# Expert tiles turned round: tokens held stationary for the first tile of a one-tile expert and for a third tile

## The reference

```python
# 1. recurrent attention over 768 steps -> x, 1536 tokens of 384
# 2. h = x @ w_in (384x2048); g = max(h,0) + alpha*min(h,0); x = g @ w_out
# 3. experts: N = 1536, D = 384, E = 8, F = 1024
logits = x @ w_gate
expert_idx = np.argmax(logits, axis=1)
...
disp = np.zeros((E, capacity, D), dtype=np.float32)   # capacity 384
...
h = np.maximum(np.einsum('ecd,edf->ecf', disp, w1), 0.0)
y = np.einsum('ecf,efd->ecd', h, w2)
...
out[i] = gate_w[i] * y[expert_idx[i], pos[i]]
```

## Time and profile before

| | |
|---|---|
| median of 3 runs | 450.17 us (448.96 to 450.79) |
| the profiled execution's own time | 451.07 us |
| its span, first to last instruction | 449.2 us |
| PE busy | 423.4 us, 94% of the span |
| DVE / ACT / POOL busy | 259.4 / 197.1 / 176.4 us |
| mean granted TensorE clock | 0.983 of full speed |
| mean DMA traffic | 137 GB/s |

### The profile page before, as it was taken

One profiled execution on the slowest core, in us unless ns is written; L12 is line 12 of the kernel. 1 busy time (PEld: TensorE's weight loads), 2 busy tenths in 40 slices (PEclk: granted clock), 3 DMA queues, 4 the chain that ended last, 5 costly groups with the idle time before them and its releaser, 6 DMA issues.

```text
span 449.2 us, 9383 instructions
## 1 busy us (share of the span) xinstructions
PE 423.4 (94%) x3333; PEld 409.6 (91%) x3333; DVE 259.4 (58%) x555; ACT 197.1 (44%) x450; POOL 176.4 (39%) x189
## 2 busy tenths in 40 slices
PE   6799999999999999999999986699999999998893
PEld 5688889999999999999999985599999999998893
DVE  6798867775435333633437663444578684648820
ACT  2789943432311122111323332334568684548721
POOL 4999616553323532244535851420110311011112
PEclk9899999999999999999999998989999999999997
DMA  7996034537950000000013440683676866564000
GB/s 251 403 337 193 3 112 141 154 88 254 367 217 19 35 1 0 0 35 18 0 35 91 139 140 17 227 307 92 207 218 197 262 190 204 158 211 110 10 19 7
DMA packets 33935, 61.45 MB, mean 137 GB/s; under 512 B 4654, under 2 KB 26910, under 8 KB 33888
## 3 DMA queue, kind: packets, MB, share of 16 engines
q1 hardware_dynamic: 31008, 55.53, 38.4%
q0 software_dynamic: 2880, 5.29, 3.4%
HBM read 47.53 MB, written 14.79 MB: 139 GB/s over the span
## 4 chain that ended last, share of the span: by engine, by line
PE 79%; DVE 7%; ACT 5%; issue 3%; POOL 2%; DMA 2%; POOLq 0%; SPq 0%; DVEq 0%; ACTq 0%
PE bank L1150 20%; PE bank L1165 19%; PE bank L1275 18%; PE bank L1304 14%; ACT scores L611 3%; PE bank L1262 2%; PE bank L1119 1%; PE bank L1083 1%; ACT w_high L594 1%; DVE scores L826 1%; DMA xe<-routed_rows 1%; DVE neg L884 1%; DVE act_full L890 1%; PE bank L1111 1%; PE bank L1069 1%
## 5 line engine op out<-in xcount | busy, mean ns | idle before, releaser
L510 POOL TENSOR_TENSOR g_low<-act_full,g_high 128x384 fp32r<-128x384 f32 x63 | 63.8, 1012 | 114.5 <-ACT g_high L640 114.5
L640 ACT ACTIVATE g_high<-act_full 128x384 fp32r<-128x384 f32 x64 | 33.7, 526 | 150.0 <-DVE act_full L890 137.3
L1150 PE MATMUL bank<-x_split,w_high 128*128 (+1 forms) x384 | 98.4, 337 | 0.0
L884 DVE TENSOR_SCALAR neg<-bank,alpha_sb 128x384 f32<-128x384 f32 x64 | 39.2, 613 | 71.5 <-PE bank L1150 71.4
L566 POOL DMA_INDIRECT out<-y_out,token x24 | 25.2, 1049 | 124.6 <-ACT y_out L727 123.4
L1150 PEld LDWEIGHTS bank<-x_split,w_high 128*128 128x128 f32 x384 | 69.0, 188 | 0.2 <-issue 0.2
L1165 PE MATMUL bank<-w_high,g_high 128*128 128x384 f32 x189 | 65.1, 344 | 1.2 <-POOL g_low L510 1.2
L1150 PE MATMUL bank<-x_split,w_low 128*128 (+1 forms) x192 | 64.4, 336 | 0.0
L1165 PE MATMUL bank<-w_high,g_low 128*128 128x384 f32 x189 | 63.8, 337 | 0.0
L1165 PE MATMUL bank<-w_low,g_high 128*128 128x384 f32 x189 | 63.7, 337 | 0.0
L1275 PE MATMUL bank<-xe_high,w_high 128*128 128x256 f32 (+1 forms) x192 | 58.8, 306 | 1.6 <-DVE xe_low L1003 1.6
(11 more groups left out here) (127 smaller groups left out, 796.2 us busy)
## 6 DMA issues: line engine op xcount, KB each, us to landing
w_raw<-chunks SPq DMA_DIRECT2D x96, 192.0 KB, 3.3
w_raw<-chunks SPq DMA_DIRECT2D x32, 384.0 KB, 3.2
rk_in<-att_rk SPq DMA_DIRECT2D x12, 704.0 KB, 6.3
routed_rows<-fill SPq DMA_DIRECT2D x1, 5211.0 KB, 17.3
xe<-routed_rows SPq DMA_DIRECT2D x7, 579.0 KB, 5.5
v_in<-att_v SPq DMA_DIRECT2D x12, 200.0 KB, 5.5
out<-fill SPq DMA_DIRECT2D x1, 2304.0 KB, 23.4
x_split<-x_split POOLq DMA_DIRECT2D x18, 48.0 KB, 2.6
```

The lines of the kernel that those rows point to most:

```text
L510: pool.tensor_tensor(gl[:, f % 4, :], act_full[:, f % 2, :], gh[:, f % 4, :].bitcast(f32), ALU.subtract).then_inc(s_gl, 1)
L640: act.activation(gh[:, f % 4, :], act_full[:, f % 2, :], ACT.Copy).then_inc(s_gh, 1)
L884: dve.tensor_scalar(neg[:, f % 2, :], h, 0.0, alpha_sb[:, f:f + 1], ALU.min, ALU.mult)\
L1150: last = mm(bank[f % 4][:, 0:G], a[:, f, w], x[:, kc, bass.ds(g * G, G)], start=kc == 0 and i == 0, stop=kc == KC - 1 and i == 2)
```

## The change

An expert now has two branches of its own on PE and one on ACT and DVE.

- *One tile* (`rows[e] < P + 1`): `flip_up` holds the tile of tokens stationary and streams four weight blocks at once, 9 matmuls of 512 columns for half of the hidden units, into bank 0 or 1. `flip_relu` (DVE) writes the maximum with 0 into the new buffer `gn`, `flip_turn` (PE) transposes it block by block into bank 2 or 3, `flip_high` (ACT) and `flip_low` (DVE) make `egh` and `egl`. The turns of the next expert's three tiles stand between the two halves.
- *Otherwise*: up with 256 columns, then down of tile 1.
- *A third tile*: `flip_up` and so on for tile 2 alone, between the halves of tile 0's down part; its down part comes last.
- DVE and ACT run `flip_relu`, `flip_high` and `flip_low` for tile 2 in every expert, also where there is none; PE then has released them in advance. PE's next use of banks 0 to 3 waits for them (`flip_banks_free`).
- The second halves of the weights are split in one run behind the up part; the output tiles are copied in the order 1, 2, 0 (`Y_ORDER`), tile 0 behind all eight splits of first halves.
- Expert 0 starts with two turned tiles; the third is turned after block 1. Chunks 29 to 31 are split between its blocks. SP waits for expert 0's rows before it issues further loads.

```diff
@@ -417,6 +426,8 @@
             sp.wait_ge(s_scat, 16 * T)
             for i in range(GT):
                 sp.dma_start(xe[:, 0, i, :], disp[i * P:(i + 1) * P, :]).then_inc(s_xe0[i], 16)
+            for i in range(GT):
+                sp.wait_ge(s_xe0[i], 16)
             for m in range(DEFER, RAW):
                 load_chunk(2 * NF - RAW + m, m)
             load_xe(1)
...
-                pool.wait_ge(s_yo, e * GT + GT - i + C_YO)
+                pool.wait_ge(s_yo, e * GT + Y_ORDER.index(i) + 1 + C_YO)
...
+            for e in range(E):
+                for i in Y_ORDER:
+                    y_scatter(e, i, s_out if e < E - 1 else s_last)
+                if e < E - 1:
+
+                    pool.wait_ge(s_out, (e + 1) * 16 * GT)
+                    pool.sem_inc(s_gone, 1)
...
-                act.wait_ge(s_mh, (e - FIRST) * NFE + f + 1)
+                act.wait_ge(s_w1free, e - FIRST + 1)
...
-            for i in range(GT):
+            for i in range(GT - 1):
                 xe_high(0, i, bank[4 + i])
-            for c in range(2 * NF - 3, 2 * NF):
-                split_high(c)
...
+            def flip_high(e, i):
+
+                act.wait_ge(s_step, e * NFE + FFN_STEPS)
+                act.wait_ge(s_yd[2], e)
+                for half in range(2):
+                    act.wait_ge(s_ft[i // 2], 2 * e + half + 1)
+                    if i:
+                        act.wait_ge(s_mgl, e * NFE + NFE + C_MGL)
+                    act.activation(egh[:, half * HF:(half + 1) * HF, i * P:(i + 1) * P],
+                                   bank[2 + half][:, :].rearrange("p (f n) -> p f n", f=HF), ACT.Copy)\
+                       .then_inc(s_fc[i // 2], 1)
+
+            for e in range(E):
+                with act.If(rows[e] < P + 1):
...
+                    if e < E - 1:
+                        for i in range(GT):
+                            xe_high(e + 1, i, bank[4 + GT - 1 - i])
+                    flip_high(e, 0)
+                    act.sem_inc(s_mgh, NFE)
+                with act.Else():
+                    act.sem_inc(s_fc[0], 2)
+                    for f in range(NFE):
+                        relu(e, f, 2 * P)
+                        if e == 0 and f == 1:
+                            xe_high(0, 2, bank[6])
+                        if e == 0 and 3 <= f < 6:
+                            split_high(2 * NF - 6 + f)
+                        if f in TURN and e < E - 1:
+                            xe_high(e + 1, TURN[f], bank[4 + GT - 1 - TURN[f]])
+                if FIRST <= e + 1 < E:
+                    for f in range(NFE):
                         split_high2(e + 1, f)
-
-            for e in range(E):
-                with act.If(rows[e] < 2 * P + 1):
-                    ups(e, 2 * P)
-                with act.Else():
-                    ups(e, CAP)
+                y_copy(e, 1)
+                flip_high(e, 2)
                 for f in range(NFE):
                     if e + FIRST < E:
                         split_high1(e + FIRST, f)
-                    if f in (3, 5, 7):
-                        y_copy(e, (7 - f) // 2)
+                    if f == HF:
+                        y_copy(e, 2)
+                y_copy(e, 0)
...
+            def flip_relu(e, i, half):
+
+                dve.wait_ge(s_fh[i // 2], 2 * e + half + 1)
+
+                if i:
+                    dve.wait_ge(s_ft[0], 2 * e + 2)
+                elif e:
+                    dve.wait_ge(s_ft[1], 2 * e)
+                dve.tensor_scalar(gn[:, half * HF * P:(half + 1) * HF * P], bank[half][:, :], 0.0, None, ALU.max)\
+                   .then_inc(s_fr[i // 2], 1)
+
+            def flip_low(e, i, half):
+                dve.wait_ge(s_fc[i // 2], 2 * e + half + 1)
+                part = (slice(0, P), slice(half * HF, (half + 1) * HF), slice(i * P, (i + 1) * P))
+                op = dve.tensor_tensor(egl[part], bank[2 + half][:, :].rearrange("p (f n) -> p f n", f=HF),
+                                       egh[part].bitcast(f32), ALU.subtract)
+                if i:
+                    op.then_inc(s_fl, 1)
+                else:
+                    op.then_inc(s_mgl, HF)
...
+            for e in range(E):
+                with dve.If(rows[e] < P + 1):
+                    flip_relu(e, 0, 0)
...
+                    if e < E - 1:
+                        for i in range(GT):
+                            xe_low(e + 1, i, bank[4 + GT - 1 - i])
+                    flip_relu(e, 0, 1)
+                    for half in range(2):
+                        flip_low(e, 0, half)
+                with dve.Else():
+                    dve.sem_inc(s_fr[0], 2)
+                    for f in range(NFE):
+                        relu_low(e, f, 2 * P)
+                        if e == 0 and f == 1:
+                            xe_low(0, 2, bank[6])
+                            keep_meta(0)
+                        if e == 0 and 3 <= f < 6:
+                            split_low(2 * NF - 6 + f)
+                        if f in TURN and e < E - 1:
+                            xe_low(e + 1, TURN[f], bank[4 + GT - 1 - TURN[f]])
+                if FIRST <= e + 1 < E:
...
                         split_low2(e + 1, f)
-
-            for e in range(E):
-                with dve.If(rows[e] < 2 * P + 1):
-                    ups(e, 2 * P)
-                with dve.Else():
-                    ups(e, CAP)
                 if e < E - 1:
                     keep_meta(e + 1)
+                for half in range(2):
+                    flip_relu(e, 2, half)
+                for half in range(2):
+                    flip_low(e, 2, half)
                 if e + FIRST < E:
                     for f in range(NFE):
                         split_low1(e + FIRST, f)
...
+                if e == 1 and i == 0:
+                    pe.wait_ge(s_tel, GT)
+
                 xe_there(pe, e, (i,))
                 for kc in range(KC):
                     last = pe.transpose(dst[:, kc * P:(kc + 1) * P], xe[:, e % 2, i, kc * P:(kc + 1) * P], ident[:, :])
                 last.then_inc(s_te, 1)
+
+            def flip_banks_free(e, b):
+
+                if b < 2:
+                    pe.wait_ge(s_fr[1], 2 * (e - 1) + 1 + b)
+                else:
+                    pe.wait_ge(s_fl, 2 * (e - 1) + b - 1)
+
+            def y_bank_free(e, i):
+
+                pe.wait_ge(s_yo, (e - 1) * GT + Y_ORDER.index(i) + 1 + C_YO)
...
+                if e and f < 4:
+                    flip_banks_free(e, f)
...
+                    if e == 0 and f == 1:
+                        turn_xe(0, 2, bank[6])
...
+            def expert_down(e, i, fs=range(NFE)):
+
+                if fs[0] == 0:
+                    turned(e, i)
...
-                    pe.wait_ge(s_mgl, s + 1 + C_MGL)
+                    if i == 2:
+
+                        pe.wait_ge(s_fl, 2 * e + f // HF + 1)
+                    else:
+                        pe.wait_ge(s_mgl, s + 1 + C_MGL)
...
+            def no_tile(e, i):
+
+                turned(e, i)
+                pe.sem_inc(s_yd[i], 1)
+
+            def flip_up(e, i, half):
+
+                slot = e * NFE % SLOTS + half * HF
+                w1_ready(pe, e, half * HF + HF - 1)
                 if i:
-                    last.then_inc(s_yd[i], 1)
+                    pe.wait_ge(s_tel, e * GT + GT)
+
+                    pe.wait_ge(s_mgl, e * NFE + HF + half + 1 + C_MGL)
+                elif e:
+                    pe.wait_ge(s_mgl, (e - 1) * NFE + HF + half + 1 + C_MGL)
+                    flip_banks_free(e, half)
+                for kc in range(KC):
+                    for m, (x, w) in enumerate(((xeh, wh), (xeh, wl), (xel, wh))):
+                        last = mm(bank[half][:, :].rearrange("p (f n) -> p f n", f=HF),
+                                  x[:, e % 2, kc, i * P:(i + 1) * P], w[:, slot:slot + HF, kc * P:(kc + 1) * P],
+                                  start=kc == 0 and m == 0, stop=kc == KC - 1 and m == 2)
+                last.then_inc(s_fh[i // 2], 1)
+
+            def flip_turn(e, i):
+
+                for half in range(2):
+                    pe.wait_ge(s_fr[i // 2], 2 * e + half + 1)
+                    if i:
+
+                        pe.wait_ge(s_mgl, e * NFE + NFE + C_MGL)
+                    elif e:
+                        pe.wait_ge(s_mgl, e * NFE + C_MGL)
+                        flip_banks_free(e, 2 + half)
+                    for k in range(HF):
+                        f = half * HF + k
+                        last = pe.transpose(bank[2 + half][:, k * P:(k + 1) * P], gn[:, f * P:(f + 1) * P], ident[:, :])
+                    last.then_inc(s_ft[i // 2], 1)
 
             pe.wait_ge(s_g, FFN_STEPS)
             keep_warm(2 * WARM)
@@ -1318,24 +1450,43 @@
 
             pe.wait_ge(s_scat, 16 * T)
             keep_warm(8 * WARM)
-            for i in range(GT):
+            for i in range(GT - 1):
                 turn_xe(0, i, bank[4 + i])
 
             for e in range(E):
```

(81 more changed lines are left out.)

33 lines of the change are left out of this document (19 added, 14 removed).

## The result

The changed kernel takes 452.94 us (450.62 to 454.02, 9 runs) where the one before takes 450.17 (448.33 to 450.79): ratio 1.0067, interval 1.0051 to 1.0084. It is slower, by more than this kernel's noise. The forecast was 445.0, and 448.0 was the end of its range. The profiled execution took 452.98 us.

What follows compares the result with a forecast made beforehand. PE, busy 94% of the span, plus its waits was taken as the bound. Terms -0.2 +1.1 +0 -4.0 -1.3 -0.9 = -5.3 took the median 450.17 to 444.9; 0.1 for latencies gave 445.0, range 442.5 to 448.0.

Steps and rivals of the forecast that it cites:

- the end of a one-tile expert: Expert 5's down part, once its low part is done: 24 matmuls at 0.173, 4.16 us, ending at 11.2.
- 0.45 each as in rows 2: Branches not hidden in three experts, 0.45 us each, giving 446.4; part of a rival with chance 0.20.
- The rival for more waits and a fall of the clock: Expert 6 or 7: more waits or one more clock fall, costing up to 1.5 us, 446.5; chance 0.20.
- Third tiles: Experts 0 and 4: separate 512-column matmuls and eight transposes for the third tile cost +1.1 us an expert.
- Experts 1 to 3: Two-tile experts: same matmuls, 1.8 us of slack for ACT's work, priced 0.
- Expert 5: First one-tile expert: takes 11.2 us instead of 15.2, saving 4.0, with 1 us of waits left.
- Expert 6's waits: PE idle three times, for DVE's empty maximum, `y_copy` and DVE again; expert takes 14.0 us, saving 1.3.
- Expert 7: Last one-tile expert: waits 1.7 us for the empty maximum, takes 11.9 instead of 12.8, saving 0.9.
- SP's wait: Loads for experts 1 and 2 held until 288.80, at most 4.5 us later: priced 0, at most 1.
- Start of expert 0: Products begin at 289.4 instead of 290.98, -1.6 us; 0.2 saved over the whole expert.
- The clock at expert 0: Half-clock loss of 1.5 us at expert 0 kept; rival that the clock stays up: 443.5, chance 0.24.

Runs made afterwards that it cites:

- swap: Changed kernel with jumps kept, the larger side of each branch written first on PE, ACT and DVE: 447.14 us, ratio 0.9948 to the kernel before.
- s_nospwait: static2 without SP's wait for expert 0's rows: 445.15 us, ratio 0.9902 to the kernel before.
- static2: Changed kernel with fixed tile counts in place of every run-time test on PE, ACT and DVE: 447.07 us, ratio 0.9953 to the kernel before.
- s_oldstart: static2 with the whole start of the kernel before put back, without SP's wait: 446.23 us, ratio 0.9933 to the kernel before.
- before_static2: Kernel before the change, with fixed tile counts in place of its run-time tests: 448.74 us, ratio 0.9983 to the kernel before.
- swap_rest: Changed kernel with the larger side written first on ACT and DVE alone, PE as changed: 452.71 us, ratio 1.0080 to the kernel before.
- warm2: Changed kernel, jumps kept, with dummy transposes filling PE's waits in experts 5 to 7: 453.11 us, ratio 1.0079 to the kernel before.
- best: swap without SP's wait and with the empty third tile's flip skipped in the one-tile side: 443.15 us, ratio 0.9851 to the kernel before.
- static_warm2: Changed kernel with both fixed tile counts and dummy transposes in PE's waits: 446.69 us, ratio 0.9939 to the kernel before.

## Why the prediction was wrong

**The step that failed** is the one on the end of a one-tile expert: "when the down part starts: 24 x 0.173 = 4.16". It took a down part to run at its pitch once its operand is there, and jumps to be free or, in a rival, "0.45 each as in rows 2". That 0.45 was read where nothing had to be fetched late. A jump over a side of some hundred matmuls held up TensorE's instructions for 2.5 to 3.8 us; with a nearly empty queue it cost PE 1.8 and 1.2 us in experts 6 and 7, and the half clock behind it adds some 1.9 over both. Taken together that is 1.2% or 5.4 us, from `swap` against the changed kernel: it alone turns the forecast gain of 5.2 into nothing. The rival for more waits and a fall of the clock had the right place and was sized at 1.5 us.

**Other steps.**
- *Third tiles* +1.1 an expert: right (27.11 against 25.96), and with it the pitch of 512 columns.
- *Experts 1 to 3* free: right. PE was busy in 53.82 of 53.82 us.
- *Expert 5*, 11.2: measured 11.9. The walk took 0.2 from a matmul to its reader and nothing at the engines' start; PE waited 0.35 and 0.80 at the two places. A small mis-sizing.
- *Expert 6's waits* (1.2, about 1.1, about 1.6 foreseen, 3.9 in all): 0.83, 0.64, 1.33 measured. The causes are right, the sizes a little large. Without gaps of fetching, in `swap`, expert 6 takes 16.1 us (411.46 to 427.54) and not 14.0. Most of it is the clock, which falls there after all: ten matmuls or so at 0.32, 1.6 us, which was in a rival. About half a microsecond is the start of the down part: 0.53 of issue stands behind the last transposes, where the walk had 0.2 in all.
- *Expert 7*: the 1.7 us wait ahead of it didn't come, since expert 6's down part had got longer; in `swap` it takes 10.8.
- *SP's wait* "priced 0, at most 1": the reason given was that the first load is used 5 us later and lands in 3.3. But the load that was late was that of expert 1's rows, which stands behind the others and took 6.58. It cost 0.55 in the profiled run and about 2 us by `s_nospwait` against `static2`.
- *Start of expert 0*: 1.6 foreseen. From the first turn to the first product it went from 4.11 us (286.87 to 290.98) to 2.80 (287.42 to 290.22 in PE's timeline of the changed kernel), so 1.3 were won there. In the profiled run 0.55 of them went into SP's wait; by the medians the new start with that wait is worth nothing, as `s_oldstart` shows:

```profile
287.42 0.82 PE L1336 MATMUL bank<-ident,xe 128*128 128x128 f32 x6
290.22 0.36 PE L1362 MATMUL bank<-xe_high,w_high 128*128 128x256 f32 x1 [1.98 <-DVE xe_low L1037]
```

- *The clock at expert 0* did not fall, which was the second likeliest case. It brought little against the median. It isn't the new start that keeps the clock up: in `before_static2`'s trace, with the old start, it didn't fall there either, and in `swap_rest`'s, with the new one, it was at half from 290.0 to 293.4. So the fall in the earlier trace rows was probably one of that execution.

The sum for the miss of 8.2 us (1.0067 against 0.9885): 5.4 for TensorE's jumps, up to 1.6 for the clock in expert 6 that still falls in `swap`, about 1 to 2 for SP's wait. These overlap, since a shorter wait also keeps the clock up; they are not independent terms. The first and the third are each measured on a pair of kernels that differ in nothing else; the clock's part is not.

## What to carry to other kernels

When a branch makes an engine's path shorter, ask what it has queued when it jumps. Here a jump over some hundred matmuls held the instructions up for 2.5 to 3.8 us. Behind 24 queued matmuls, 4.2 us of work, that was hidden or cost up to 1.2 us, by how far the engine had got; behind a wait it cost 1.2 to 1.8. Writing the long side first, so that the short path jumps at its start and not ahead of its last part, gave back 1.2% without touching any work. Work on empty tiles costs its full time on the engine that the short path waits for; a semaphore increment in its place is enough.

## What was not expected of the hardware

- An issue gap can stand some instructions behind the jump that causes it: behind the first matmul of the down part in expert 6, behind the fifth in expert 7, and both come back at their places in `swap_rest` (1.68 and 1.63).
- The trace can name another engine for a late instruction. In `warm2` and `best` the same kind of gap was put down to a weight split (2.28 and 1.16 us).
- With dummy 128x128 transposes of the identity in PE's waits the granted clock stayed at full in experts 5 to 7 (`warm2`, `static_warm2`). It isn't shown that they did it, for it stayed at full in `s_nospwait` without them.
- The clock in expert 6 is on an edge. `static2` waits there for 0.89, 0.63 and 1.34 us and falls to half behind them; `s_nospwait` waits for 0.87, 0.65 and 1.33 and stays at full. A window of each behind its down part's start:

```profile
422.30:425.70 3.40, 3.40 (x13) 3.40 (x12) 3.40 (x9) 3.40 (x9) 0.00 (x0) 0.50 0.00 0
```

```profile
420.80:424.20 3.40, 3.40 (x21) 3.23 (x19) 3.40 (x9) 3.40 (x9) 0.00 (x0) 1.00 0.00 0
```

So up to 1.6 us of a difference between two of these kernels can be the clock's, and isn't theirs.
